# One-core linear attention, ELU feed-forward and dense experts: the low parts of the weight slices divided anew between two engines, and a diagonal instead of a product for chunks 2 and 3

## The reference

```python
def _attn_ref(r, k, v, w, u):            # B 2, H 8, S 768, D 48
    state = np.zeros((B, H, D, D))
    for t in range(S):
        cur = np.einsum('bhd,bhe->bhde', u[None] * kt, vt)
        y[:, :, t] = np.einsum('bhd,bhde->bhe', rt, state + cur)
        state = wt[:, :, :, None] * state + np.einsum('bhd,bhe->bhde', kt, vt)

h = x @ w_in                             # x 1536x384, w_in 384x2048, w_out 2048x384
g = np.where(h > 0.0, h, np.exp(np.minimum(h, 0.0)) - 1.0)
x = g @ w_out

p = domain_probs / (domain_probs.sum(-1, keepdims=True) + 1e-09)
for e in range(4):                       # w1[e] 384x1024, w2[e] 1024x384
    out += p[:, e:e + 1] * (np.maximum(x @ w1[e], 0.0) @ w2[e])
```

## Time and profile before

| | |
|---|---|
| median of the runs | 656.65 us |
| the profiled execution | 656.64 us |
| its span, first to last instruction | 654.8 us |
| PE busy | 649.4 us (99%), 4661 matmuls |
| DVE busy | 392.2 us (60%) |
| ACT busy | 239.8 us (37%) |
| POOL busy | 247.3 us (38%) |

### The profile page before, as it was taken

How to read it: one execution, slowest core, us unless ns; L and a number is a source line. 1 busy time by engine, 2 the same in 40 slices (tenths; PEclk the granted TensorE clock), 3 DMA queues, 4 the chain that set the end, 5 groups by cost and what they waited for, 6 DMA issues and landing times.

```text
span 654.8 us, 12678 instructions
## 1 busy us (share of the span) xinstructions
PE 649.4 (99%) x4661; PEld 596.8 (91%) x4661; DVE 392.2 (60%) x725; ACT 239.8 (37%) x553; POOL 247.3 (38%) x300
## 2 busy tenths in 40 slices
PE   8999999999999999999999999999999999999998
PEld 6999999877778888999999999999999999999997
DVE  7888877666434333656565656565656565656563
ACT  4786655554445444322222222222222222222221
POOL 4898423122040099993008920009910019000000
PEclk9999999999999999999999999999999999999999
DMA  8923224200000133100013100012100011001011
GB/s 330 404 107 118 87 90 162 72 21 0 2 1 1 49 98 96 49 2 2 1 34 111 49 1 0 0 49 98 49 1 0 0 49 48 1 2 48 0 49 49
DMA packets 13279, 38.08 MB, mean 58 GB/s; under 512 B 1968, under 2 KB 4016, under 8 KB 13232
## 3 DMA queue, kind: packets, MB, share of 16 engines
q1 hardware_dynamic: 12944, 37.03, 16.0%
q10 hardware_dynamic: 288, 0.39, 0.2%
HBM read 35.06 MB, written 2.36 MB: 57 GB/s over the span
## 4 chain that ended last, share of the span: by engine, by line
PE 92%; POOL 4%; issue 1%; DVE 1%; DMA 0%; ACT 0%; DVEq 0%; POOLq 0%; ACTq 0%
PE bank L1218 29%; PE bank L1219 29%; PE bank L1220 29%; POOL w_lo L503 4%; PE bank L1068 1%; PE bank L1138 1%; PE bank L1091 1%; PE bank L1150 1%; PE bank L1079 1%; DMA rkw<-rkw_dram 0%; DVE fr L781 0%; PE bank L1158 0%; PE bank L1154 0%; POOL tok L472 0%; DVE tok L799 0%
## 5 line engine op out<-in xcount | busy, mean ns | idle before, releaser
L1218 PE MATMUL bank<-x_lo,w_hi 128*128 128x256 f32 (+2 forms) x432 | 146.0, 338 | 0.6 <-POOL w_lo L503 0.6
L1220 PE MATMUL bank<-x_hi,w_hi 128*128 128x256 f32 (+2 forms) x432 | 143.4, 332 | 0.0
L1219 PE MATMUL bank<-x_hi,w_lo 128*128 128x256 f32 (+2 forms) x432 | 143.2, 331 | 0.0
L1219 PE MATMUL bank<-w_hi,g_lo 128*128 128x384 f32 x384 | 129.6, 337 | 0.0
L1220 PE MATMUL bank<-w_hi,g_hi 128*128 128x384 f32 x384 | 129.3, 337 | 0.0
L1218 PE MATMUL bank<-w_lo,g_hi 128*128 128x384 f32 x384 | 129.0, 336 | 0.0
L734 ACT ACTIVATE g_hi<-bank 128x512 fp32r<-128x512 f32 x96 | 57.6, 600 | 144.1 <-DVE bank L998 122.2
L1218 PEld LDWEIGHTS bank<-x_lo,w_hi 128*128 128x128 f32 x432 | 81.2, 188 | 10.0 <-issue 0.8
L1220 PEld LDWEIGHTS bank<-x_hi,w_hi 128*128 128x128 f32 x432 | 81.2, 188 | 9.0
L1219 PEld LDWEIGHTS bank<-x_hi,w_lo 128*128 128x128 f32 x432 | 81.3, 188 | 8.3
L515 POOL TENSOR_TENSOR raw<-raw 128x128 f32<-128x128 f32 x16 | 7.5, 468 | 200.2 <-DMA raw<-w_dram 200.2
(11 more groups left out here) (114 smaller groups left out, 1146.6 us busy)
## 6 DMA issues: line engine op xcount, KB each, us to landing
raw<-w_dram SPq DMA_DIRECT2D x48, 384.0 KB, 3.6
rkw<-rkw_dram SPq DMA_DIRECT2D x10, 772.5 KB, 5.4
tok<-tok_dram SPq DMA_DIRECT2D x10, 576.0 KB, 6.1
out_dram<-acc SPq DMA_DIRECT2D x10, 192.0 KB, 1.9
rkw<-rkw_dram SPq DMA_DIRECT2D x2, 512.0 KB, 4.3
rkw<-rkw_dram SPq DMA_DIRECT2D x2, 260.5 KB, 3.2
tok<-tok_dram SPq DMA_DIRECT2D x2, 192.0 KB, 5.0
out_dram<-acc ACTq DMA_DIRECT2D x2, 192.0 KB, 2.0
```

The lines of the kernel that those rows point to most:

```text
L1218: pe.matmul(out, wh, ml, start=start, stop=False, skip_group_check=shared)
L1219: pe.matmul(out, wl, mh, start=False, stop=False, skip_group_check=shared)
L1220: return pe.matmul(out, wh, mh, start=False, stop=stop, skip_group_check=shared)
```

## The change

Four edits; the first three lie in the first 64 us.

1. The low parts are divided by halves. DVE gets (3, 1), (13, 0) and (13, 1) besides its five slices: (3, 1) between `elu(3)` and `lo_g(3)`, (13, 0) after `lo_g(11)`, (13, 1) after `lo_g(12)`. The halves (14, 0) and (14, 1), which stood after `lo_g(12)` and `lo_g(14)`, stand after `lo_g(13)` and `lo_g(14)`.
2. POOL loses these three halves, six pieces.
3. Chunks 2 and 3 get their bonus by a diagonal, as chunk 4 and later ones do: POOL does `bonus_diagonal` in place of `bonus_v`, PE loses `turn_bonus` for them, and DVE masks by L822's instruction.
4. DVE's `bonus(c)` of all chunks from 2 on stands at the end of step 4c-1, behind `lo_g`; before it stood behind `elu`, in step 4c for chunks 2 and 3 and in step 4c-1 for the others.

```diff
-LO_VECTOR = (2, 5, 8, 10, 14)
-LO_POOL = (0, 1, 3, 4, 6, 7, 9, 11, 12, 13, 15)
-LO_BETWEEN = {1: (5, 0), 2: (5, 1), 4: (8, 0), 5: (8, 1), 6: (10, 0), 7: (10, 1)}
-LO_AFTER = {12: (14, 0), 14: (14, 1)}
+LO_BETWEEN = {1: ((5, 0),), 2: ((5, 1),), 3: ((3, 1),), 4: ((8, 0),), 5: ((8, 1),), 6: ((10, 0),), 7: ((10, 1),)}
+LO_AFTER = {11: ((13, 0),), 12: ((13, 1),), 13: ((14, 0),), 14: ((14, 1),)}
...
-SUMS_OF_BONUS = {c: step - 1 if c >= DIAGONAL else step for c, step in SCORES.items()}
...
-            if n in LO_VECTOR:
-                eng.wait_ge(s_wv, LO_VECTOR.index(n) * 2 + part + 1)
+            if (n, part) in LO_VECTOR:
+                eng.wait_ge(s_wv, LO_VECTOR.index((n, part)) + 1)
...
             pool.wait_ge(s_qp, FIRST)
-            lo_w(0)
-            lo_w(1)
-            lo_w(3)
-            lo_w(4)
-            lo_w(6)
-            lo_w(7)
+            before = [LO_POOL.index(half) for half in ((9, 0), (9, 1), (15, 0))]
+            lo_ws(LO_POOL[:before[0]])
             bonus_terms(2)
-            lo_w(9)
-            bonus_v(2)
-            lo_w(11)
-            lo_w(12)
+            lo_ws(LO_POOL[before[0]:before[1]])
+            bonus_diagonal(2)
+            lo_ws(LO_POOL[before[1]:before[2]])
             bonus_terms(3)
-            lo_w(13)
-            bonus_v(3)
-            lo_w(15)
-            for c in range(DIAGONAL, NC):
+            bonus_diagonal(3)
+            lo_ws(LO_POOL[before[2]:])
+            for c in range(4, NC):
                 bonus_terms(c)
                 bonus_diagonal(c)
...
                 elu(n)
-                for c in due(n, 0, SUMS_OF_BONUS):
-                    bonus(c)
...
+                for c in due(n, -1):
+                    bonus(c)
+                for half in LO_AFTER.get(n, ()):
+                    lo_w(*half)
                 for c in due(n, 0, PRODUCTS):
                     products(c)
...
                 up(bank[bank_of(n)][:, 0:width(n)], tokens(t), j, n == 0)
-                for c in due(n, 2):
-                    if c < DIAGONAL:
-                        turn_bonus(c, BESIDE["yt"])
                 if n >= LAG:
                     down1(n - LAG)
```

More of the change, by code:

```diff
@@ L90 @@
 NUPDATE = NC - B
-LO_VECTOR = (2, 5, 8, 10, 14)
-LO_POOL = (0, 1, 3, 4, 6, 7, 9, 11, 12, 13, 15)
-LO_BETWEEN = {1: (5, 0), 2: (5, 1), 4: (8, 0), 5: (8, 1), 6: (10, 0), 7: (10, 1)}
-LO_AFTER = {12: (14, 0), 14: (14, 1)}
+LO_BETWEEN = {1: ((5, 0),), 2: ((5, 1),), 3: ((3, 1),), 4: ((8, 0),), 5: ((8, 1),), 6: ((10, 0),), 7: ((10, 1),)}
+LO_AFTER = {11: ((13, 0),), 12: ((13, 1),), 13: ((14, 0),), 14: ((14, 1),)}
+LO_VECTOR = [(2, 0), (2, 1)] + [half for step in range(J1) for half in LO_BETWEEN.get(step, ()) + LO_AFTER.get(step, ())]
+LO_POOL = [(n, half) for n in range(J1) for half in range(2) if (n, half) not in LO_VECTOR]
 STRIP = 32
 STRIPS = DM // STRIP
-PIECES = 4
+PIECES = 2
 HI_FIRST = 6
@@ L102 @@
               11: ((14, 0), (14, 1)), 12: ((15, 0),), 13: ((15, 1),)}
-DIAGONAL = 4
-SUMS_OF_BONUS = {c: step - 1 if c >= DIAGONAL else step for c, step in SCORES.items()}
 HI_HALVES = [half for step in sorted(HI_BETWEEN) for half in HI_BETWEEN[step]]
@@ L294, in slice_ready @@
         def slice_ready(eng, n, part):
-            if n in LO_VECTOR:
-                eng.wait_ge(s_wv, LO_VECTOR.index(n) * 2 + part + 1)
+            if (n, part) in LO_VECTOR:
+                eng.wait_ge(s_wv, LO_VECTOR.index((n, part)) + 1)
             else:
-                eng.wait_ge(s_wq, LO_POOL.index(n) * PIECES + (part + 1) * (PIECES // 2))
+                eng.wait_ge(s_wq, (LO_POOL.index((n, part)) + 1) * PIECES)
         def slot_of(e, j):
@@ L329, in diagonal_done @@
         def diagonal_done(c):
-            return 2 * (c + 1 - DIAGONAL)
+            return 2 * (c + 1 - FIRST)
         def bonus_done(eng, c):
-            if c >= DIAGONAL:
+            if c >= FIRST:
                 eng.wait_ge(s_diag, diagonal_done(c))
@@ L476, in bonus_terms @@
                     pool.tensor_tensor(t[:, r], t[:, r], u_rep[:, r], ALU.mult).then_inc(s_rk, 1)
[L478 to L484, removed]
             def bonus_diagonal(c):
@@ L494, in bonus_diagonal, with lo_w @@
                                        channel_multiplier=-1).then_inc(s_diag, 1)
-            def lo_w(n):
+            def lo_w(n, half):
+                pool.wait_ge(s_wh, hi_done(n, half))
                 for i in range(PIECES):
[L499 to L502, removed]
+                    need(pool, s_wq, LO_POOL.index((n, half)) * PIECES + i)
+                    first = half * DM + i * (DM // PIECES)
+                    part = slice(first, first + DM // PIECES)
                     pool.tensor_tensor(w_lo[:, n, part], raw[:, n, part], w_hi[:, n, part].bitcast(F32),
@@ L565, in _, with lo_ws @@
             pool.wait_ge(s_qp, FIRST)
-            lo_w(0)
-            lo_w(1)
-            lo_w(3)
-            lo_w(4)
-            lo_w(6)
-            lo_w(7)
+            def lo_ws(halves):
+                for half in halves:
+                    lo_w(*half)
+            before = [LO_POOL.index(half) for half in ((9, 0), (9, 1), (15, 0))]
+            lo_ws(LO_POOL[:before[0]])
             bonus_terms(2)
-            lo_w(9)
-            bonus_v(2)
-            lo_w(11)
-            lo_w(12)
+            lo_ws(LO_POOL[before[0]:before[1]])
+            bonus_diagonal(2)
+            lo_ws(LO_POOL[before[1]:before[2]])
             bonus_terms(3)
-            lo_w(13)
-            bonus_v(3)
-            lo_w(15)
-            for c in range(DIAGONAL, NC):
+            bonus_diagonal(3)
+            lo_ws(LO_POOL[before[2]:])
+            for c in range(4, NC):
                 bonus_terms(c)
@@ L817, in mask_scores @@
                 found = banks["x"][o][:, :].rearrange("p (a t) -> p a t", a=PAIRS)
-                if c < DIAGONAL:
+                if c < FIRST:
                     dve.tensor_tensor(att[:, o, :, :], found, masks, ALU.mult).then_inc(s_att, 1)
@@ L939, in _ @@
                 elu(n)
-                for c in due(n, 0, SUMS_OF_BONUS):
-                    bonus(c)
                 if n == 0:
                     add_update(0, BANKS0)
-                if n in LO_BETWEEN:
-                    lo_w(*LO_BETWEEN[n])
+                for half in LO_BETWEEN.get(n, ()):
+                    lo_w(*half)
                 past = n // J1 - 1
@@ L962, in _ @@
                     add_update(1, BANKS1)
-                if n in LO_AFTER:
-                    lo_w(*LO_AFTER[n])
+                for c in due(n, -1):
+                    bonus(c)
+                for half in LO_AFTER.get(n, ()):
+                    lo_w(*half)
                 for c in due(n, 0, PRODUCTS):
@@ L1120, in turn_bonus @@
                 pe.wait_ge(s_cv, c + 1)
-                if c >= FIRST:
-                    y_free(c)
                 for k in range(KT):
@@ L1132, in old_values @@
                 pe.wait_ge(s_st, PAIRS * (c - 1))
-                if c >= DIAGONAL:
-                    y_free(c)
+                y_free(c)
                 q = q_of(c)
@@ L1138, in old_values @@
                     pe.matmul(strip_of(yt, b), st[:, c % 2, p, first:first + STRIP], q[:, p * CH:(p + 1) * CH],
-                              start=c >= DIAGONAL and b < P // STRIP, stop=True, skip_group_check=True)
+                              start=b < P // STRIP, stop=True, skip_group_check=True)
             def values_even(c, yt):
```

## The result

The changed kernel takes 661.96 us, the median of six runs (661.50 to 662.61), against 656.65 us before: a ratio of 1.0082 (95% interval 1.0071 to 1.0092), 5.3 us slower. The forecast was 659.2 us with a range up to 661.2.

The account below looks back on a forecast made before the run. PE's own list of matmuls was taken to bound the kernel before 64 us. The wait before `up(14)`, +2.90, less 0.33 for the second transposes gave +2.57: 656.65 + 2.6 = 659.2 us, range 657.9 to 661.2.

Parts of the forecast that it names:

- What bounds the kernel: Before 64 us PE's own matmuls bound: every us taken from PE's path shortens the kernel, every us waited lengthens it.
- What goes from PE: Waits before `up(9)` and `up(13)`, 0.44 and 0.61 us, and two transpose groups, 0.33 each, go: 1.7 us won, were that all.
- The wait before `up(14)`: Step 14: PE waits for DVE's (14, 0) behind `lo_g(13)`; `up(14)` starts at 57.56 instead of 54.66, +2.90 us.
- The clock: Rival: PE's clock falls in the hole before `up(14)`, costing 3.1 us, giving 662.3 us; chance 0.15.
- (3, 1) in step 3: DVE's 0.55 us half falls in a 0.66 us gap before `lo_g(3)` and costs nothing; +0.6 at most if late.
- The rest: Later sums move behind `lo_g` by 1 to 1.4 us, covered by 2.9 us at chunk 4; nothing lost.
- the rival in which the half is ready in time: Before `up(14)`: (14, 0) ends by 53.3 us, so waits and transposes simply go: 654.9 us; chance 0.05.

Follow-up runs that it names:

- the last version: Changed kernel with (13, 0) and (14, 0) on DVE ahead of chunk 3's sum, (13, 1) and (14, 1) on POOL behind (15, 0): 655.08 us.
- the one move on the kernel before: Kernel before with only (14, 0) moved from behind `lo_g(12)` to behind `lo_g(13)`: two runs at 658.95 and 658.98 us, two at 660.41 and 660.59.
- the kernel with the hole filled: Changed kernel with 34 matmuls, their results overwritten, on PE between `down(11)` and `up(14)`: 659.88 us.
- the sum of chunk 3: Changed kernel with the sum of chunk 3 alone back behind `elu(12)`: 658.79 us once, and 660.20, 660.26 and 660.41.
- the first experiment: Changed kernel with (14, 0) and (13, 1) exchanged, so DVE makes (14, 0) behind `lo_g(12)` and (13, 1) behind `lo_g(13)`: 656.62 us, ratio 1.0001.
- the diagonals alone: Kernel before with diagonals for chunks 2 and 3, their sums in step 4c-1 behind `elu`, low parts unchanged: 657.90, 657.97, 657.99, 659.08 and 660.51 us.
- the halves alone: Kernel before with the changed kernel's division of low parts by halves; products, transposes and sums as before: 661.39 us.

## Why the prediction was right in kind and wrong in size

*What bounds the kernel.* Right for losses: what is lost ahead of 60 us stays lost, the shift of 5.22 at `up(15)` is 5.26 in the time of the profiled executions (661.90 - 656.64). Wrong for gains: "every us taken from PE's path before 64 us shortens the kernel by itself" does not hold. With the halves exchanged PE led by 1.37 us at `up(15)` and by nothing at `up(19)`, since DVE could not follow.

*What goes from PE.* Right but for 0.37 us. The distance before `up(9)` is 0.41 (0.41 forecast), the one before `up(13)` 0.64 (about 0.5), and `up(13)` starts at 51.45 instead of 52.46, where 51.08 was wanted: 0.23 of that is what is left of the wait for (13, 0), 0.16 comes from `down(4)` (below). The second group of transposes is worth the 0.33. Once DVE is relieved as well, the gain of 1.7 is nearly to be had: the last version has 1.5.

*The wait before `up(14)`.* Right in place, releaser and cause, shown by the exchange of the two halves and by the one move on the kernel before. The term was mis-sized: +2.90 forecast, +3.61 measured. Three pieces make up the 0.71 (they come to 0.79, and 0.08 was won in between). POOL's terms of chunk 3 ended at 50.25, not 49.95, so `elu(12)` started at 51.22 instead of the 50.99 of the earlier trace rows (+0.23). From the start of (13, 1) to the scan it took 0.87 us instead of 0.46 (+0.41), as the half lasted 0.94 and not 0.55. The rest is the way from the end of the half to PE's first matmul, 58.12 to 58.27 (+0.15). All else that DVE did there came within 0.1. The idle time of PE was 4.6 us (53.65 to 58.27) where 4.3 was forecast.

*The clock.* This is the step that failed: the sum put the fall of the clock at nothing, and it took 1.9 us. With the mis-sized wait alone the sum is 659.2 + 0.7 = 659.9, inside the range, and 659.88 is what the kernel with the hole filled takes. The prediction named the rival and its place, and then gave it 0.15, on the ground that waits of 0.44 and 0.61 us had left the clock alone. Such waits say nothing about a hole seven to ten times as long. In the six runs of the changed kernel it fell every time (0.995 five times, 0.997 once). The rule cited from the Trainium skill ("TensorE: Matmul & The Clock Gate", section "Why this matters for your kernels") was the better witness here, though not for each single execution: behind 3.7 us of waiting (the sum of chunk 3) the clock stood once in four. With 659.2 + 1.9 + 0.7 for the mis-sized wait the sum is 661.8, against 661.96. The range ended at 661.2, short of what happened in six runs of six.

That the rival's own 662.3 came so near is luck. Its 3.1 us were taken from the opening matmuls, over which the trace of before gives a granted clock of 1.00 (0 to 8 us), and nothing ties their length to that of a fall. It was 1.2 too dear, and the wait 0.7 too short.

*(3, 1) in step 3* was hidden, as said, but the scan behind it took 1.67 us instead of 1.49 beside POOL's shifted pieces, and `down(4)` started 0.16 us later against the start of `up(0)`. The wait before `up(14)` ate that.

*The rest.* The sums and diagonals from chunk 4 on cost nothing, as forecast; no wait for them shows up after 60 us in the changed kernel. That DVE with its new halves has no slack from step 12 to 15 and takes PE's lead back there was not in the prediction. It did not matter for the changed kernel, but it would have spoilt the rival in which the half is ready in time: that one comes out at 656.62 (the first experiment), not at 654.9.

## What to carry to other kernels

When work moves in a hand-written order, ask of each consumer not only on which engine its input now is made, but behind which result of the consumer's own last group it stands; a half put behind `lo_g(13)` made PE wait for a round trip through itself. Price a hole in PE's work twice, by its length and by the clock at which PE comes back, and if the trace has no hole of that length, do not let short waits vouch for it. And where an engine waits for another ahead of one instruction, put there what depends on neither.

## What the runs showed of the hardware

The fall of the clock is not a function of the program alone. I count a run as fallen when its mean granted clock is 0.997 or 0.995; all others have 0.999 or 1.000. The waits are those of the profiled executions; in the other runs only the mean clock is known, and that the fall lies behind the same wait is inferred. With PE waiting 2.2 us (the single move) it fell in two runs of four, with 2.3 us (the diagonals alone) in two of five, with 3.7 us (the sum of chunk 3) in three of four, with 3.8 us (the halves alone) in five of five and with 4.5 us (the changed kernel) in six of six. It never fell in the 43 runs of the four versions without such a hole, nor in the four runs with the hole filled. So one profile at clock 1.000 does not clear a kernel whose PE waits 2 us: the times of the same program then scatter by 1.1 to 2.6 us, where those of the versions without a hole agree within 0.3.

The price differs from run to run too, and the mean clock tells it: 0.997 cost 1.5 us in the single move (658.97 to 660.5 us) and 1.1 with the diagonals alone (657.97 to 659.08), where 0.995 cost 2.5 (660.51); 0.995 cost 1.1 us more than 0.997 with the halves alone (662.4 against 661.3) and 0.5 more in the changed kernel (662.0 against 661.5).

The same half of 128x384 takes DVE 0.55 us or up to 1.00, and POOL's work beside it does not yet make the difference: both the short one of the kernel before (0.55 at 52.20) and the long one of the changed kernel (0.94 at 52.42) lie beside POOL's pieces. POOL's piece before, then in the changed kernel:

```profile
51.73 0.59 POOL L503 TENSOR_TENSOR w_lo<-raw,w_hi 128x192 fp32r<-128x192 f32 x1
```

```profile
52.36 0.59 POOL L492 TENSOR_TENSOR w_lo<-raw,w_hi 128x192 fp32r<-128x192 f32 x1
```

The first ends at 52.32, 0.12 us after DVE's half has begun; the second at 52.95, 0.53 after. In the traces of the 11 kernels, 76 such halves start while an instruction of POOL still has more than 0.15 us to run; 75 of them end 0.41 to 0.42 us after that instruction (one took 0.55 all the same), and the other 54 halves take 0.54 to 0.57. So the length of the half goes with how much of POOL's instruction is left when DVE comes to it, and the 0.41 us by which (13, 1) was mis-sized depend on when POOL's piece began. The Trainium skill ("GPSIMD Engine Reference", section "Specifications") states that POOL's SBUF interfaces are shared with DVE, with contention when a DVE instruction has two SBUF inputs, as these subtractions have. The ends above agree with that; that the interface is the cause was not tested by itself.
